# The routing's gate inside the mixer: three tiles at once, with the gate weights as stationary operand

## What is computed

```python
# mixer, per batch and head, for t in sequence
m_new = max(f[t] + m, i[t])
C = exp(f[t] + m - m_new) * C + exp(i[t] - m_new) * outer(v[t], k[t])
n = exp(f[t] + m - m_new) * n + exp(i[t] - m_new) * k[t]
y[t] = sigmoid(o[t]) * (C @ q[t]) / max(abs(n @ q[t]), 1)
# routing over x = y as 3072 rows of 320
logits = x @ w_gate                      # 3072 x 8
for idx in argsort(-logits.flatten()):   # greedy, each expert takes 384 rows
    ...
# expert e: relu(x[mask] @ w1[e]) @ w2[e]; then elu(x @ w_in) @ w_out
```

## Time and profile before

| | us |
|---|---|
| median of 3 runs | 837.94 (837.02 to 840.19) |
| profiled execution | 841.97 |
| its span, first to last instruction | 840.3 |
| TensorE busy in the span | 95% |
| VectorE, ScalarE, GpSimd busy | 62%, 56%, 47% |
| mixer | about 18 to 182 us |
| routing and experts | from 182 us to the end |

### The profile page before, as it was taken

One profiled execution on the slowest core, in us unless ns is written; L12 is line 12 of the kernel. 1 busy time (PEld: TensorE's weight loads), 2 busy tenths in 40 slices (PEclk: granted clock), 3 DMA queues, 4 the chain that ended last, 5 costly groups with the idle time before them and its releaser, 6 DMA issues.

```text
span 840.3 us, 17700 instructions
## 1 busy us (share of the span) xinstructions
PE 794.3 (95%) x6029; PEld 741.3 (88%) x6029; DVE 524.4 (62%) x1438; ACT 466.6 (56%) x990; POOL 392.7 (47%) x466
## 2 busy tenths in 40 slices
PE   5999999989979999999999999999999999999994
PEld 5899999987768889899989989998999899999894
DVE  5566776766768567665866585576658656542441
ACT  5445545422417663785478276728835772893672
POOL 3535454454623652465076345516552662664133
PEclk9999999999999999999999999999999999999998
DMA  4999999413410212111122201121211212121000
GB/s 78 142 154 178 151 169 171 100 57 112 124 53 26 84 48 68 46 55 55 44 69 62 69 26 60 48 68 47 71 55 45 69 48 68 47 70 39 2 1 23
DMA packets 137987, 60.96 MB, mean 73 GB/s; under 512 B 104696, under 2 KB 136184, under 8 KB 137912
## 3 DMA queue, kind: packets, MB, share of 16 engines
q1 hardware_dynamic: 135608, 52.13, 28.7%
q0 software_dynamic: 2304, 7.87, 2.9%
HBM read 51.67 MB, written 8.26 MB: 71 GB/s over the span
## 4 chain that ended last, share of the span: by engine, by line
PE 63%; DVE 9%; ACT 3%; issue 1%; POOL 1%; DMA 0%; ACTq 0%; POOLq 0%
PE bank L1825 7%; PE bank L1910 7%; PE bank L1826 6%; PE bank L1828 6%; PE bank L1912 6%; PE bank L1911 6%; PE bank L1830 3%; PE bank L1829 3%; PE bank L1868 3%; PE bank L1866 3%; PE bank L1867 3%; PE bank L1762 2%; DVE cmp L849 2%; DVE unit L1506 2%; DVE unit L1503 2%
## 5 line engine op out<-in xcount | busy, mean ns | idle before, releaser
L1243 POOL TENSOR_TENSOR gl_lo<-unit,gl_hi 128x384 fp32r<-128x384 f32 x128 | 130.3, 1018 | 274.3 <-ACT gl_hi L1700 274.2
L1910 PE MATMUL bank<-Wo_hi,gl_hi 128*128 128x320 f32 x384 | 125.6, 327 | 0.5 <-POOL gl_lo L1243 0.5
L1912 PE MATMUL bank<-Wo_hi,gl_lo 128*128 128x320 f32 x384 | 119.3, 311 | 0.0
L1911 PE MATMUL bank<-Wo_lo,gl_hi 128*128 128x320 f32 x384 | 119.2, 310 | 0.0
L1503 DVE SCALAR_TENSOR_TENSOR unit<-bank,unit 128x384 f32<-128x384 f32 x104 | 57.8, 555 | 84.2 <-ACT bank L1693 79.3
L1664 ACT ACTIVATE hid_hi<-bank 128x384 fp32r<-128x384 f32 x64 | 31.4, 491 | 127.5 <-PE bank L1830 127.5
L1681 ACT ACTIVATE unit<-bank 128x384 f32<-128x384 f32 x128 | 62.2, 486 | 62.8 <-PE bank L1830 53.5
L1825 PE MATMUL bank<-x_hi,Wi_hi 128*128 128x384 f32 x224 | 81.3, 363 | 2.4 <-DVE unit L1506 1.6
L1826 PE MATMUL bank<-x_hi,Wi_lo 128*128 128x384 f32 x224 | 76.6, 342 | 0.0
L1910 PEld LDWEIGHTS bank<-Wo_hi,gl_hi 128*128 128x128 f32 x384 | 73.2, 191 | 3.1 <-POOL gl_lo L1243 3.1
L1506 DVE TENSOR_TENSOR unit<-unit,bank 128x384 f32<-128x384 f32 x128 | 70.9, 554 | 4.4
(11 more groups left out here) (289 smaller groups left out, 2125.6 us busy)
## 6 DMA issues: line engine op xcount, KB each, us to landing
stage<-in_moe_w_dram SPq DMA_DIRECT2D x32, 320.0 KB, 2.9
stage<-in_moe_w_dram SPq DMA_DIRECT2D x32, 256.0 KB, 2.6
stage<-in_moe_w_dram SPq DMA_DIRECT2D x96, 64.0 KB, 2.4
k_in<-in_k_dram SPq DMA_DIRECT2D x24, 160.0 KB, 3.6
q_in<-in_q_dram SPq DMA_DIRECT2D x24, 160.0 KB, 4.2
o_in<-in_o_gate_dram SPq DMA_DIRECT2D x24, 160.0 KB, 4.1
v_in<-in_v_dram SPq DMA_DIRECT2D x24, 160.0 KB, 3.6
x_rows<-xt SPq DMA_DIRECT2D x24, 160.0 KB, 3.3
```

The costliest lines, as they stand in the source:

```text
L1243: nc.gpsimd.tensor_tensor(gl_lo[:, b, :], ex[:, b, :], gl_hi[:, b, :].bitcast(F32), ALU.subtract).then_inc(gl_ok, 1)
L1910: nc.tensor.matmul(acc[j][:, 0:DM], gl_hi[:, f % RG, t_], Wo_hi[:, f, :], start=(f == 0), stop=False)
L1911: nc.tensor.matmul(acc[j][:, 0:DM], gl_hi[:, f % RG, t_], Wo_lo[:, f, :], start=False, stop=False)
L1912: ins = nc.tensor.matmul(acc[j][:, 0:DM], gl_lo[:, f % RG, t_], Wo_hi[:, f, :], start=False, stop=(f == NF2 - 1))
```

## The change

What it does, by engine:

- TensorE: the gates of tiles 0 to 20 go. Instead, in each body with u = 2 from tile 5 on (seven of them), `gate_three` works on the three tiles g - 5 to g - 3 whose xT lie in the ring: for each of the three pieces of the model dimension and each tile one matmul with 32 columns of gate weights as stationary operand and xT (128 columns) as the moving one. Tile j's result lies in partitions 32j to 32j + 31 of columns 384 to 511 of bank 7. It stands where the gate stood and waits for `scaled` of tile g - 1. After the products, `gate_turned` transposes the 128 x 128 result, back into the same columns.
- ScalarE: in these bodies a copy of the 96 rows out of the bank into the new tile `by_expert`, before the copy of xT.
- VectorE: one copy of 3 x 8 columns into L for the three tiles, between the wait for the scores and PW. The waits for the gate ahead of `state` and the single copies go. `carried` of the next body waits for this copy.
- The gates of the last three tiles (21 to 23) stay as they were, behind the loop.
- The key transposes no longer wait for the logits' copy. GpSimd clears `by_expert` at the start.

```diff
+        by_expert = sb("by_expert", [P, P])
+        pG = bank[7][:, H * VP:H * VP + P]
+        def three_beside(g, u):
+            return u == RING - 1 and not (peeled(g) and g < RING)
...
             nc.gpsimd.memset(wg[:], 0.0)
+            nc.gpsimd.memset(by_expert[:], 0.0)
...
+            def logits_of_three(g, i):
+                dve.wait_ge(turned_pe, i)
+                nc.vector.tensor_copy(L[:, bass.ds(g - 2, RING), :],
+                                      pG[:, 0:RING * SLOT].rearrange("p (g e) -> p g e", g=RING)[:, :, 0:E]).then_inc(lg_ok, RING)
+
@@ VectorE, body
-                if not (peeled(g) and g < 3):
-                    dve.wait_ge(lg_pe, g - 2)
                 if last:
                     state(*last)
-                if not (peeled(g) and g < 3):
-                    logits(g - 3)
-                if last:
                     summed(*last)
                 dve.wait_ge(s_pe, g + 1)
+                if three_beside(g, u):
+                    logits_of_three(g - 3, i)
@@ ScalarE, body
+                if three_beside(g, u):
+                    act.wait_ge(three_pe, i)
+                    nc.scalar.copy(by_expert[0:RING * SLOT, :], pG[0:RING * SLOT, :]).then_inc(three_ok, 1)
@@ TensorE, gather_in and carried
-                if not (peeled(g) and g < 4):
-                    pe.wait_ge(lg_ok, g - 3)
...
+                if three_beside(g, u):
+                    pe.wait_ge(lg_ok, i * RING)
@@ TensorE, the new functions
+            def gate_three(b, c):
+                g, u, i = tile_of(b, c)
+                pe.wait_ge(xt_ok, g - RING + 1)
+                if peeled(g) and g < 2 * RING:
+                    pe.wait_ge(wg_in, 48)
+                pe.wait_ge(fin_step, g * 6 - 5)
+                for n in range(3):
+                    for j in range(RING):
+                        ins = nc.tensor.matmul(pG[j * SLOT:(j + 1) * SLOT, :], wg[:, n, 0:SLOT], xT[j][:, n, :], start=(n == 0), stop=(n == 2))
+                ins.then_inc(three_pe, 1)
+
+            def gate_turned(i):
+                pe.wait_ge(three_ok, i)
+                nc.tensor.transpose(pG, by_expert[:], ident[:]).then_inc(turned_pe, 1)
@@ TensorE, body
-                if not (peeled(g) and g < 3):
-                    gate(g - 3, u, g)
+                if three_beside(g, u):
+                    gate_three(b, c)
                 if last:
                     products(*last)
+                if three_beside(g, u):
+                    gate_turned(i)
```

More of the change, by code:

```diff
@@ L162, in build @@
         lg_ok = sem("lg_ok")
+        three_pe = sem("three_pe")
+        three_ok = sem("three_ok")
+        turned_pe = sem("turned_pe")
         x_stored = [sem(f"x_stored{u}") for u in range(RING)]
@@ L479, in state @@
                 ins.then_inc(c_ok, 1)
+            def logits_of_three(g, i):
+                dve.wait_ge(turned_pe, i)
+                nc.vector.tensor_copy(L[:, bass.ds(g - 2, RING), :],
+                                      pG[:, 0:RING * SLOT].rearrange("p (g e) -> p g e", g=RING)[:, :, 0:E]).then_inc(lg_ok, RING)
             def logits(g):
-                dve.wait_ge(lg_pe, g + 1)
+                dve.wait_ge(lg_pe, g - (G - RING) + 1)
                 nc.vector.tensor_copy(L[:, bass.ds(g, 1), :].rearrange("p o e -> p (o e)"), pL[:, 0:E]).then_inc(lg_ok, 1)
@@ L707, in gate @@
                 pe.wait_ge(kt_ok, newest + 1)
[L708 to L711, removed]
+                pe.wait_ge(lg_ok, g)
                 for n in range(3):
```

## The result

| | before | changed kernel |
|---|---|---|
| median, us | 837.61 (837.02 to 840.19) | 846.36 (843.94 to 849.67) |
| ratio | | 1.0101, 95% interval 1.0053 to 1.0149 |
| profiled execution, span | 841.97, 840.3 | 844.15, 842.4 |
| first experts' matmul (end of the mixer) | 182.56 | 187.01 |

Both medians are of four runs; the 837.94 stated ahead of the prediction is that of three of them.

The account below looks back on a forecast made before the run. TensorE's issue order was taken to bound the mixer. Terms -14.1 + 9.1 + 9.6 + 0.45 = +5.1 us, plus 3.0 for the clock, on 837.94 gave 846.0 us; 8-in-10 range 840.5 to 851.5.

Parts of the forecast that it names:

- The wait: TensorE before the new gate, until VectorE has scaled the previous tile's products: seven waits, 9.6 us in all.
- The new gate: Nine matmuls on TensorE in seven bodies: 0.99 us plus 0.2 for tiling changes; with 0.11 for the turned transpose, 9.1 in all.
- Rival 3: New gate's three column groups run fully side by side: 843.7 us with two clock falls, 840.7 with none; chance 0.11.
- The old gates: Tiles 0 to 20 in the mixer lose their gate on TensorE: 21 x 0.67 = 14.1 us off the path.
- The end: After the last scores, the last carried products wait for VectorE's copy of the logits: 0.45 us.
- ScalarE's copy: Copy of 96 rows x 128 columns out of the bank: some 0.3 us, hidden while ScalarE is idle.
- The sum without the clock: Mixer terms together: -14.1 + 9.1 + 9.6 + 0.45 = +5.1 us.
- The clock: TensorE's granted clock falls after two of the seven new stalls, 1.5 us each: +3.0 us (0 to 7.5).
- Rival 1: The stall without the clock: no fall behind the new gaps, 843.0 us; chance 0.20.
- Rival 2: Nothing overlaps in the new gate's column groups: 6.9 us more, 853 with two falls, 850 without; chance 0.12.
- rival 4: Transfers pace the mixer, hiding TensorE's savings and stalls; only the end's 0.45 us stays: 838.4 us; chance 0.08.
- rival 5: Faster: VectorE's scaling is early enough, so 4.5 us are gained: 833.4 us; chance 0.04.

Follow-up runs that it names:

- experiment 8: Kernel before with each tile's old gate issued twice: 861.66 us, ratio 1.0275 to the kernel before.
- experiments 1: The "wait alone": kernel before, old gates kept, TensorE given the new wait for the scaling in the seven bodies: 852.81 us against 838.64, ratio 1.0166.
- the other order: Changed kernel with the new gate's nine matmuls ordered tile by tile, one column group after another: 847.55 us.

## Why the prediction was right

The forecast was 846.0, the measurement 846.36 (+8.1 and +8.75 on the medians of before), and the mechanism was the one that it named. Step by step:

- **The wait.** Forecast 0.76, 1.13 and 2.06 us; measured 0.78, 1.21, and 2.05 twice. Only the first gap at c = 5 was mis-sized, 2.72. The prediction held that the two chains start from the same scores and that what TensorE saves earlier can't change their difference; here it did. VectorE was still adding the products when the scores were there, since its work had filled the shorter body, and reached PW 0.2 us later. And `xt` took twice its time beside GpSimd's masking. That the two engines block each other is read from timelines, not tested: `xt` takes 0.96 or 0.97 us wherever the masking began at most 0.02 us ahead of it (in seven traces), and 0.49 where `xt` was first. Sum 10.4 instead of 9.6.
- **The new gate** was mis-sized the other way: 0.79 us with all changes of tiling, forecast 0.99 + 0.2. I had taken the scores' 0.11 for a matmul as the price of alternating groups; with groups of columns it is 0.066. Rival 3 (0.66, plus the changes) was nearer, and so was the Trainium skill's speedup for column groups (TensorE: Matmul & The Clock Gate, Part 3), 0.83 as an estimate. That is 7 x 0.4 = 2.8 us less.
- **The old gates**, 0.67 each: as forecast, by traces and by experiment 8.
- **The end**: 0.51 for 0.45. **GpSimd's clearing**: forecast nothing; TensorE's second wait ended 0.18 us later (14.10 to 14.28), the upper bound.
- **ScalarE's copy** took 0.26 us, and nobody waited for it.
- **The sum without the clock**: forecast +5.1, by measured parts -14.1 + 6.3 + 10.4 + 0.5 = +3.1.
- **The clock**: forecast two falls at 1.5 us, +3.0. The first trace had none behind a gap in the mixer, the second two that cost 4.8, and filling three gaps gave 4.05 back. By the clocks of all runs it is 3.3 to 4.8 us, about half of the loss.

So the total was as good as this by luck, as errors cancelled: the parts without the clock came out 2.0 us cheaper, the gate above all, and the clock, with what the parts leave open, dearer by 2.6. Rival 1 was what the first trace showed, with a cheaper gate; the median holds the falls. Rival 2 (no overlap) is out by the 0.79 us, rival 4 (transfers) by experiments 1 and 8, rival 5 by the gaps.

## What to carry to other kernels

When work moves to another bank, ask who reads that bank at that moment: seven waits cost 10.4 us, more than the 7.8 that the exchange of 21 matmul groups for seven wider ones gave. A wait on a saturated TensorE is priced by laying both engines' chains from their common start side by side, and by asking what unrelated operation stands in the other chain; here a 1.38 us comparison did. Moving it took the loss away, and using another bank's free columns made the change a gain of 0.5%. Add the clock's risk to gaps of 1 to 3 us, the sizes behind which it fell here, and compare the mean granted clocks of many runs before a single trace is taken for the whole.

## What was not expected of the hardware

- The granted clock fell in or just behind gaps of 1.0 to 2.7 us in some executions and not in others of the same kernel: after three of six gaps of 1.0 to 1.6 us in the experts of before, and after seven of twelve of 2.0 to 2.7 us in the mixer (none and two of three in the two traces of the changed kernel, two of three in the other order, three of three in the wait alone). The six traces without such a gap in the mixer have no fall between 41 and 182 us. A fall cost 1.6 us, once 3.2.
- The start of the mixer varies with the clock too. Up to the scores of tile 3 kernel before and "wait alone" run the same instructions, and reached them at 41.79 and 45.28 us; the second had the clock at 0.50 for most of 25 to 34 us:

```profile
28.00:32.00 4.00, 4.00 (x25) 3.83 (x26) 0.50 (x1) 0.47 (x1) 1.50 (x2) 0.50 0.68 147
```

- An fp32 record of 32 stationary and 128 moving columns costs 0.06 us in one column group and 0.03 us with three groups alternating, against 0.11 for one of 128 stationary and 96 moving columns.
